# Scores in one place from slot 46, five banks for the turns and batch 0's mixing, its low-rank sum in PSUM, and the MLP from slot 56

## The chip, the cores and the metric

The kernel runs on one core of a Trainium2 chip. The metric is the device time of one execution in microseconds (us). Instructions are named by engine: TensorE (PE), VectorE (DVE), ScalarE (ACT), GpSimd (POOL) and SyncE (SP), which issues DMAs. Each engine takes its own instructions in order and waits on semaphores.

## The reference

Attention over 4 batches, 8 heads, 576 positions and head size 64, with rotary positions, is followed by a token mixing of rank 32 and an MLP over channels, everything in float32.

```
scores = (rot(q) @ rot(k).T) / sqrt(64)
attn   = exp(scores - max) / (sum + 1e-9)
x      = attn @ v                       # (4, 576, 512), heads side by side
u      = x + V.T @ (U.T @ x)            # over positions, rank 32
out    = u + relu(u @ w_ch1) @ w_ch2    # 512 -> 2048 -> 512
```

## The kernel before

**Number format.** Matmuls run in a rounded float32 format. To keep precision an operand is split into a rounded upper half and the rest (pth and ptl, xh and xl, uth and utl, hth and htl, w1h and w1l), and the products of the halves are summed. ScalarE makes the upper halves, VectorE or GpSimd the rest.

**Slots.** Work goes in slots n, one for each tile of scores (160 tiles: 32 heads of 5 tiles, the fifth with 64 rows), and 17 slots more. All engines walk through the same slots; the order in each is written out by hand. In slot n TensorE makes the scores of tile n (L881), VectorE their negated row maximum (L743), ScalarE the exponential (L606). TensorE then transposes ("turns") exponentials of earlier tiles into PSUM (L908 for the tail keys, L915 for the rest, five small ones for a head's last tile), ScalarE rounds them into pth or, for a head with its buffer there, into uth (L617), VectorE writes the rest (L752, L756). The product with v of head g-1 (L895) runs in two halves, in slots that `pv_of` gives; ScalarE copies its lower part to low (L623), VectorE adds it into xt (L766).

**Mixing.** `MIX_ALONE` says in which slot of the next batch's stretch each step of batch 0's mixing is put (s = n - 40), `MIX_MERGED` the same for the others. Steps are: natural (x turned back and scaled: L927 TensorE, L790 VectorE, then ScalarE's xh L631 and GpSimd's xl L526), low (U times x, two matmuls L937 and L938 into a bank, which VectorE copies, L803, or adds, L806, into hsum), hidden (ScalarE copies hsum to hs, L636; VectorE the rest, L810), residual (L943, VectorE L814), turned_u (L949, ScalarE L641, VectorE L818).

**MLP.** Steps of an up product (two parts of six matmuls, L967) and a down product (three parts of three matmuls, L985) are given to slots by `parts_by_slot`, from costs in the code, so that each of the `REGIONS` has a fixed number of parts. The first two steps' weights are rounded at slot `PRIME` (L648) and their rests made by GpSimd (L532); SyncE loads the first three steps' weights at slot PRIME - 3. What is left after the last slot follows in one run.

**Two orders.** Up to slot `MERGED` = 59 the mixing of slot n is done in slot n by TensorE, and in slot n + 1 by VectorE and ScalarE; scores alternate between banks 0-1 and 2-3. From slot 59 all engines do slot n's work in slot n, scores have one place (banks 0-1), so TensorE's scores wait for the exponential of the slot before, banks 2 to 4 gather the down products, bank 5 is the up product's, and turns, products with v and mixing share banks 6 and 7. Before slot 59 these share the ring of banks 4 to 7. `bank_plan` hands out banks in the order of the work; whoever takes a bank waits until the last tenant has been read (`_release`). From slot `EARLY` = 52 turns follow their scores by one slot, before by two.

## Time and profile before

| | us |
|---|---|
| median of 3 runs | 784.0 (782.77 to 784.78) |
| profiled execution | 786.62 |
| its span | 784.8 |
| TensorE busy | 716.6 |
| VectorE busy | 407.5 |
| ScalarE busy | 439.2 |
| GpSimd busy | 461.2 |

The span runs from the first to the last instruction of the profile. Busy time counts an instruction from its start to its end; matmuls overlap their predecessors' ends, so the start-to-start distance is a matmul's price in a stream. Line numbers are those of the kernel above. A slot begins on TensorE with four matmuls of L881.

### The profile page before, as it was taken

What the parts mean: (1) busy time and instruction counts of PE and PEld (TensorE: products, weight loads), DVE (VectorE), ACT (ScalarE), POOL (GpSimd) and SP (SyncE); (2) the same over time, 40 slices, a digit from 0 to 9 for tenths busy, and PEclk for the clock granted to TensorE, in tenths of its full rate; (3) what the DMA queues carried; (4) which work ended last, traced back from release to release, by engine and by line L of the source; (5) the groups of instructions that cost most, each with busy time, mean ns of one, the idle gap of its engine ahead of it and who ended that gap; (6) DMA issues with size and microseconds to landing.
All of it is one profiled execution on the core that took longest, in us unless ns stands there. A gap on an engine that the chain in (4) does not pass through costs nothing.

```text
span 784.8 us, 12208 instructions
## 1 busy us (share of the span) xinstructions
PE 716.6 (91%) x4252; PEld 643.5 (82%) x4252; DVE 407.5 (52%) x669; ACT 439.2 (56%) x944; POOL 461.2 (59%) x334
## 2 busy tenths in 40 slices
PE   0599988789999989999999999999999699999998
PEld 0588876579999777989898988889999579899896
DVE  2489997655555776444354456675555642112111
ACT  1578885557566665555465555666665333333332
POOL 2848867157767673485584866647523226556553
PEclk9989998989999999999999999999999999999999
DMA  7957761826474535728548266282623135445442
GB/s 224 224 145 191 197 181 61 237 102 154 160 182 174 147 115 169 233 75 204 174 140 232 92 176 178 89 235 74 175 69 119 41 128 164 133 160 167 129 162 80
DMA packets 74700, 119.59 MB, mean 152 GB/s; under 512 B 27152, under 2 KB 27280, under 8 KB 72848
## 3 DMA queue, kind: packets, MB, share of 16 engines
q1 hardware_dynamic: 73600, 116.98, 51.0%
q10 hardware_dynamic: 1040, 1.84, 0.8%
q8 instruction: 35, 0.57, 0.3%
q14 instruction: 25, 0.20, 0.1%
HBM read 81.04 MB, written 9.44 MB: 115 GB/s over the span
## 4 chain that ended last, share of the span: by engine, by line
PE 71%; DVE 10%; ACT 6%; issue 5%; DMA 4%; POOL 3%; SPq 1%; ACTq 0%; POOLq 0%; DVEq 0%
PE ps L967 23%; PE ps L985 22%; PE ps L895 8%; PE ps L881 8%; PE ps L915 6%; DVE negmax L743 2%; ACT prob L606 2%; DMA stack<-raw 1%; PE ps L908 1%; DVE ptl L752 1%; PE ps L949 1%; POOL raw L489 1%; DVE pth L756 1%; DMA tables<-in_sin 1%; DMA res<-in_v 1%
## 5 line engine op out<-in xcount | busy, mean ns | idle before, releaser
L532 POOL TENSOR_TENSOR w1l<-w1u,w1h 128x512 fp32r<-128x512 f32 x96 | 123.9, 1291 | 243.3 <-ACT w1h L648 243.2
L743 DVE TENSOR_REDUCE negmax<-ps 128x1 f32<-128x576 f32 (+1 forms) x160 | 120.4, 752 | 74.3 <-PE ps L881 71.4
L827 DVE SCALAR_TENSOR_TENSOR htl<-ps,hth 128x384 fp32r<-128x384 f32 x96 | 53.5, 557 | 191.3 <-ACT hth L659 191.2
L881 PE MATMUL ps<-stack 128*128 128x288 f32 (+1 forms) x640 | 120.5, 312 | 32.2 <-DMA stack<-raw 22.5
L606 ACT ACTIVATE prob<-ps,negmax 128x576 f32<-128x576 f32 (+1 forms) x160 | 117.9, 737 | 46.0 <-DVE negmax L743 43.3
L617 ACT ACTIVATE pth<-ps 128x512 fp32r<-128x512 f32 x162 | 90.9, 565 | 82.0 <-PE ps L915 80.2
L967 PE MATMUL ps<-uth,w1h 128*128 128x384 f32 x384 | 133.1, 347 | 0.5 <-DVE utl L818 0.5
L881 PEld LDWEIGHTS ps<-stack 128*128 128x128 f32 (+1 forms) x640 | 97.7, 185 | 43.6 <-issue 22.8
L659 ACT ACTIVATE hth<-ps 128x384 fp32r<-128x384 f32 x96 | 47.1, 491 | 150.5 <-PE ps L967 150.3
L967 PE MATMUL ps<-utl,w1h 128*128 128x384 f32 x384 | 129.8, 338 | 0.0
L967 PE MATMUL ps<-uth,w1l 128*128 128x384 f32 x384 | 129.8, 338 | 0.0
L538 POOL TENSOR_TENSOR w2l<-w2u,w2h 128x512 fp32r<-128x512 f32 x96 | 123.8, 1290 | 4.6 <-ACT w2h L652 4.6
L985 PE MATMUL ps<-w2h,hth 128*128 128x512 f32 x288 | 117.7, 409 | 2.1 <-DVE htl L827 1.2
L985 PE MATMUL ps<-w2l,hth 128*128 128x512 f32 x288 | 114.1, 396 | 0.0
L985 PE MATMUL ps<-w2h,htl 128*128 128x512 f32 x288 | 113.8, 395 | 0.0
L915 PE MATMUL ps<-ident,prob 128*128 128x128 f32 (+1 forms) x672 | 96.6, 269 | 10.5 <-DVE xt L766 4.0
L752 DVE TENSOR_TENSOR ptl<-ps,pth 128x512 fp32r<-128x512 f32 (+1 forms) x135 | 85.7, 636 | 32.6 <-ACT pth L617 30.9
L915 PEld LDWEIGHTS ps<-ident,prob 128*128 128x128 f32 (+1 forms) x672 | 76.7, 143 | 18.5 <-issue 18.4
L489 POOL TENSOR_TENSOR raw<-raw,tables 128x1152 f32<-128x1152 f32 x30 | 80.2, 2675 | 16.5 <-DVE raw L725 13.4
L895 PE MATMUL ps<-pth,v 128*128 128x288 f32 x270 | 78.8, 314 | 3.1 <-DVE utl L818 1.5
L967 PEld LDWEIGHTS ps<-uth,w1h 128*128 128x128 f32 x384 | 72.9, 190 | 4.2 <-issue 1.5
L967 PEld LDWEIGHTS ps<-utl,w1h 128*128 128x128 f32 x384 | 72.8, 190 | 2.8
(68 smaller groups left out, 1093.9 us busy)
## 6 DMA issues: line engine op xcount, KB each, us to landing
w1u<-in_w SPq DMA_DIRECT2D x96, 256.0 KB, 2.7
w2u<-in_w SPq DMA_DIRECT2D x96, 256.0 KB, 2.7
stack<-raw SPq DMA_DIRECT2D x64, 288.0 KB, 4.5
raw<-in_qk SPq DMA_DIRECT2D x14, 1152.0 KB, 5.5
stack<-raw SPq DMA_DIRECT2D x60, 144.0 KB, 4.2
v2u<-in_v SPq DMA_DIRECT2D x16, 320.0 KB, 3.9
res<-scratch_u SPq DMA_DIRECT2D x18, 256.0 KB, 3.8
out<-res SPq DMA_DIRECT2D x18, 256.0 KB, 2.2
```

Of the source, the lines that this page charges most:

```text
L489: link(nc.gpsimd.tensor_tensor(both, both, tables[:, :, which], ALU.mult))
L532: nc.gpsimd.tensor_tensor(w1l[:, at], w1u[:, at], w1h[:, at], ALU.subtract).then_inc(w1_lo, 1)
L538: nc.gpsimd.tensor_tensor(w2l[:, at], w2u[:, at], w2h[:, at], ALU.subtract).then_inc(w2_lo, 1)
L606: nc.scalar.activation(tile_of(n, WT[t]).rearrange("p (c n) -> p c n", c=2), scores_of(n, WT[t]), ACT.Exp, bias=negmax[0:WT[t], t:t + 1], ...
L617: nc.scalar.activation(pt_of(g)[0][rows, keys, queries], source, ACT.Copy).then_inc(pt_hi, 1)
L743: nc.vector.tensor_reduce(negmax[0:WT[t], t:t + 1], scores_of(n, WT[t]), AX.XY, ALU.max, negate=True).then_inc(maxed, 1)
L752: nc.vector.tensor_tensor(ptl[:, :, queries], source[:, full], pth[:, full, queries], ALU.subtract).then_inc(pt_lo, 1)
L881: mm = nc.tensor.matmul(ps[0:WT[t], at + c * BANK:at + c * BANK + CH], stack[:, g % HEADS_STACKED, 0, P * t:P * t + WT[t]], stack[:, g % H ...
L895: mm = nc.tensor.matmul(work(tenant, 0, P, CH), v2[:, (g // 2) % 2, kt, g % 2], part[:, kt, CH * c:CH * c + CH], start=(kt, part) == produ ...
L915: mm = nc.tensor.transpose(bank[:, c], prob[0:rows, S * first + P * c:S * first + P * c + P], ident[0:rows, 0:rows])
L967: mm = nc.tensor.matmul(up_bank(), l[:, i % WBUF, P * d:P * d + P], r, start=(d == 0 and q == 0), stop=(d == DB - 1 and q == 2))
L985: mm = nc.tensor.matmul(acc_bank(t), l[:, i % 2, P * t:P * t + P], r[:, i % WBUF], start=(f == 0 and q == 0), stop=(f == FB - 1 and q == 2))
```

## The change

`MERGED` and `EARLY` go to 46, and a new `MLP_FROM` = 56 takes over what the MLP's start needs: the first region, `PRIME` (55) and the two-bank ring. So slots 46 to 55 run in the second order (scores in one place, mixing in its own slot on all engines) without MLP parts, with a ring of five banks, `RING_MIXED` = (4, 6, 7, 2, 3), whose count starts anew at 46. Bank 5 holds batch 0's low-rank sum: the ten matmuls of its five low steps form one accumulation, VectorE's copy and four additions for batch 0 go, and hidden reads the bank instead of hsum. The first up product waits for hidden's end instead of the last tenant of bank 5. `MIX_ALONE` is put anew over slots 46 to 57, and the products with v of heads 8 to 10 move to slots 47 and 48, 50 and 52, and 55 and 57 (before: 48 and 49, 53 and 54, 56 and 58). The first region holds the same 77 MLP parts in 37 slots.

```diff
--- before.py
+++ after.py
@@ -32,25 +32,25 @@
 LOWS = UNITS + 1
 
 
-EARLY = 52
-MERGED = 59
+EARLY = 46
+MERGED, MLP_FROM = 46, 56
 PT_TWO = 9
-PV_EARLY = {3: 0, 4: 1}
-PV_ALONE = {1: 0, 3: 1}
+PV_ALONE = {3: 0, 4: 1}
+PV_SWITCH = {2: 0, 3: 1}
 PV_MERGED = {0: 0, 2: 1}
 
-MIX_ALONE = {6: [("natural", 0)],
-             7: [("natural", 1), ("natural", 2)],
-             8: [("natural", 3)],
-             9: [("natural", 4), ("low", 0)],
-             10: [("low", 1), ("low", 2)],
-             11: [("low", 3), ("low", 4)],
-             12: [("hidden", 0)],
-             14: [("residual", 0)],
-             15: [("residual", 1), ("residual", 2)],
-             16: [("residual", 3), ("turned_u", 0)],
-             17: [("residual", 4), ("turned_u", 1), ("turned_u", 2)],
-             18: [("turned_u", 3), ("turned_u", 4)]}
+MIX_ALONE = {6: [("natural", 0), ("natural", 1)],
+             7: [("natural", 2)],
+             8: [("natural", 3), ("low", 0), ("low", 1)],
+             9: [("natural", 4), ("low", 2)],
+             10: [("low", 3), ("low", 4)],
+             11: [("hidden", 0)],
+             12: [("residual", 0)],
+             13: [("residual", 1), ("turned_u", 0)],
+             14: [("residual", 2), ("turned_u", 1)],
+             15: [("residual", 3), ("turned_u", 2)],
+             16: [("residual", 4), ("turned_u", 3)],
+             17: [("turned_u", 4)]}
 MIX_MERGED = {3: [("natural", 0)], 4: [("natural", 1), ("low", 0)], 5: [("natural", 2), ("low", 1)],
               6: [("natural", 3), ("low", 2)], 7: [("natural", 4), ("low", 3)], 8: [("low", 4)], 9: [("hidden", 0)],
               10: [("residual", 0)], 11: [("residual", 1), ("turned_u", 0)], 12: [("residual", 2), ("turned_u", 1)],
@@ -83,11 +83,11 @@
         PARTS += [("up", _i + 1, 0), ("up", _i + 1, 1)]
     PARTS += [("down", _i, _t) for _t in range(TT)]
 
-REGIONS = ((59, 93, 77), (93, 134, 237), (134, NTILES, 297), (NTILES, SLOTS, 317))
-PRIME = MERGED - 1
+REGIONS = ((56, 93, 77), (93, 134, 237), (134, NTILES, 297), (NTILES, SLOTS, 317))
+PRIME = MLP_FROM - 1
 POOL_ROUNDS = range(1, 6)
 
-RING_ALONE, RING_MERGED = (4, 5, 6, 7), (6, 7)
+RING_ALONE, RING_MIXED, RING_MERGED = (4, 5, 6, 7), (4, 6, 7, 2, 3), (6, 7)
 ACC, UP = (2, 3, 4), 5
 
 
@@ -102,7 +102,8 @@
 def pv_of(n):
 
     g, t = divmod(n, NT)
-    halves = PV_EARLY if n < NT * -(-EARLY // NT) else PV_ALONE if n < MERGED else PV_MERGED
+    first = NT * (MERGED // NT)
+    halves = PV_ALONE if n < first else PV_SWITCH if n < first + NT else PV_MERGED
     return [(g - 1, halves[t])] if 1 <= g <= NHEADS and t in halves else []
 
 
@@ -157,11 +158,16 @@
         turned = [("turned", *x) for x in turned_in(n)]
         tenants = tenants + turned if n < MERGED else turned + tenants
         tenants += [("mix", *x) for x in mixes_of(n) if x[1] != "hidden"]
-        if n == MERGED:
-            left = {b: holder[b] for b in (ACC[2], UP)}
+        if n == MLP_FROM:
+            left = {b: holder[b] for b in ACC}
+        if n in (MERGED, MLP_FROM):
             count = 0
-        ring = RING_ALONE if n < MERGED else RING_MERGED
+        ring = RING_ALONE if n < MERGED else RING_MIXED if n < MLP_FROM else RING_MERGED
         for tenant in tenants:
+            if tenant[0:3] == ("mix", 0, "low"):
+                if tenant[3] == 0:
+                    bank[tenant], before[tenant] = UP, holder.get(UP)
+                continue
             b = ring[count % len(ring)]
             count += 1
             bank[tenant], before[tenant] = b, holder.get(b)
@@ -200,7 +206,7 @@
         eng.wait_ge(e["pv_out"], 2 * i + rest[0] + 1)
     else:
         read = {"natural": "x_nat", "low": "h_sum", "residual": "u_ready", "turned_u": "ut_lo"}[rest[0]]
-        eng.wait_ge(e[read], i * NT + rest[1] + 1)
+        eng.wait_ge(e[read], i * NT + rest[1] + 1 - (NT if rest[0] == "low" else 0))
 
 
 def _down_read(eng, i, e):
@@ -306,6 +312,10 @@
          "pv_low pv_out sums_eps sums_inv nat_done x_nat x_hi x_lo x_rest low_done h_sum h_hi h_ready res_done "
          "u_ready u_stored turn_done ut_hi ut_lo w1_loaded w2_loaded w1_hi w1_lo w2_hi w2_lo up_done relu_hi "
          "relu_lo down_done acc_done added res_loaded stored").split())
+
+    def hidden_of(b):
+
+        return hsum[:, :] if b else ps[:, UP * BANK:UP * BANK + DM]
 
     def scores_of(n, rows):
         at = 2 * BANK * (n % 2 if n < MERGED else 0)
@@ -630,10 +640,12 @@
                         act.wait_ge(low_done, k - XBUF + 1)
                     nc.scalar.activation(xh[0:WT[t], k % XBUF], xn[0:WT[t], t], ACT.Copy).then_inc(x_hi, 1)
                 elif what == "hidden":
-                    act.wait_ge(h_sum, NT * (b + 1))
                     if b:
+                        act.wait_ge(h_sum, NT * b)
                         act.wait_ge(res_done, NT * b)
-                    nc.scalar.activation(hs[:, :], hsum[:, :], ACT.Copy).then_inc(h_hi, 1)
+                    else:
+                        act.wait_ge(low_done, NT)
+                    nc.scalar.activation(hs[:, :], hidden_of(b), ACT.Copy).then_inc(h_hi, 1)
                 elif what == "turned_u":
                     act.wait_ge(turn_done, k + 1)
                     if b >= 2:
@@ -794,20 +806,21 @@
                                             .broadcast_to([rows, H, D]), ALU.mult).then_inc(x_nat, 1)
                     if b == B - 1:
                         split_x(b, t)
+                elif what == "low" and b == 0:
+                    pass
                 elif what == "low":
                     dve.wait_ge(low_done, k + 1)
                     part = work(("mix", b, what, t), 0, P, DM)
                     if t == 0:
-                        if b:
-                            dve.wait_ge(h_ready, b)
+                        dve.wait_ge(h_ready, b)
                         nc.vector.tensor_copy(hsum[:, :], part).then_inc(h_sum, 1)
                     else:
-                        dve.wait_ge(h_sum, k)
+                        dve.wait_ge(h_sum, k - NT)
                         nc.vector.tensor_tensor(hsum[:, :], part, hsum[:, :], ALU.add).then_inc(h_sum, 1)
                 elif what == "hidden":
                     dve.wait_ge(h_hi, b + 1)
                     third = slice(2 * R, 3 * R)
-                    nc.vector.tensor_tensor(hs[third, :], hsum[third, :], hs[third, :],
+                    nc.vector.tensor_tensor(hs[third, :], hidden_of(b)[third], hs[third, :],
                                             ALU.subtract).then_inc(h_ready, 1)
                 elif what == "residual":
                     dve.wait_ge(res_done, k + 1)
@@ -920,7 +933,9 @@
                 if what == "hidden":
                     return
                 k, rows, tenant = b * NT + t, WT[t], ("mix", b, what, t)
-                _release(pe, before[tenant], e)
+                sums_here = b == 0 and what == "low"
+                if not sums_here or t == 0:
+                    _release(pe, before[tenant], e)
                 if what == "natural":
                     pe.wait_ge(pv_out, 2 * H * (b + 1))
                     for c in range(PAIRS):
@@ -934,9 +949,11 @@
                         pe.wait_ge(x_rest, t + 1)
                     else:
                         pe.wait_ge(x_lo, k + 1)
-                    nc.tensor.matmul(work(tenant, 0, P, DM), us[0:rows, t], xh[0:rows, k % XBUF], start=True, stop=False)
-                    mm = nc.tensor.matmul(work(tenant, 0, P, DM), us[0:rows, t], xl[0:rows, k % XBUF],
-                                          start=False, stop=True)
+                    part = hidden_of(b) if sums_here else work(tenant, 0, P, DM)
+                    nc.tensor.matmul(part, us[0:rows, t], xh[0:rows, k % XBUF],
+                                     start=not sums_here or t == 0, stop=False)
+                    mm = nc.tensor.matmul(part, us[0:rows, t], xl[0:rows, k % XBUF],
+                                          start=False, stop=not sums_here or t == NT - 1)
                     mm.then_inc(low_done, 1)
                 elif what == "residual":
                     pe.wait_ge(h_ready, b + 1)
@@ -955,7 +972,7 @@
                 if part == 0:
                     pe.wait_ge(w1_lo, i + 1)
                     if i == 0:
-                        _release(pe, left[UP], e)
+                        pe.wait_ge(h_ready, 1)
                     else:
                         pe.wait_ge(relu_lo, i)
                     if f == 0:
@@ -977,8 +994,6 @@
                 if f == 0:
                     if p:
                         pe.wait_ge(added, TT * (p - 1) + t + 1)
-                    elif ACC[t] < RING_ALONE[0]:
-                        pe.wait_ge(expd, MERGED)
                     else:
                         _release(pe, left[ACC[t]], e)
                 for q, (l, r) in enumerate(((hth, w2h), (htl, w2h), (hth, w2l))):
```

## Rows read from the trace of the kernel before

**Rows 1.** The page, its first line.
```profile
span 784.8 us, 12208 instructions
```

**Rows 2.** Windows: start:end, length, then busy us (instructions) of each engine, clock, DMA.
```profile
60.00:100.00 40.00, 38.01 (x296) 35.72 (x295) 38.21 (x66) 35.75 (x84) 33.92 (x24) 1.00 0.72 191
107.91:143.86 35.95, 28.34 (x167) 22.63 (x165) 27.29 (x47) 23.26 (x50) 19.37 (x13) 0.89 0.46 119
164.04:256.17 92.13, 92.13 (x574) 85.52 (x572) 50.45 (x85) 61.69 (x137) 66.13 (x45) 0.98 0.51 149
256.17:295.76 39.59, 35.53 (x220) 30.00 (x218) 28.22 (x44) 24.29 (x52) 27.66 (x19) 1.00 0.46 130
160.00:164.00 4.00, 1.55 (x8) 1.43 (x9) 2.31 (x5) 0.43 (x1) 1.19 (x1) 0.52 0.11 42
```

**Rows 3.** TensorE's timeline in slots 70 and 71: start, length, what.
```profile
205.30 0.40 PE L895 MATMUL ps<-pth,v 128*128 128x288 f32 x1
...
206.59 0.34 PE L967 MATMUL ps<-uth,w1h 128*128 128x384 f32 x1
...
208.68 0.69 PE L881 MATMUL ps<-stack 128*128 128x288 f32 x4
209.20 0.60 PE L915 MATMUL ps<-ident,prob 128*128 128x128 f32 x4
209.56 0.48 PE L985 MATMUL ps<-w2h,hth 128*128 128x512 f32 x1
```

**Rows 4.** TensorE's timeline, slots 46 to 60; in brackets the idle time before and its releaser.
```profile
107.91 0.77 PE L881 MATMUL ps<-stack 128*128 128x288 f32 x4
108.70 0.49 PE L915 MATMUL ps<-ident,prob 64*128 64x64 f32 x5
...
110.22 0.76 PE L881 MATMUL ps<-stack 128*128 128x288 f32 x4
...
113.57 0.77 PE L881 MATMUL ps<-stack 128*128 128x288 f32 x4
...
122.53 0.63 PE L915 MATMUL ps<-ident,prob 128*128 128x128 f32 x4 [1.30 <-DVE xt L766]
...
143.86 1.17 PE L881 MATMUL ps<-stack 128*128 128x288 f32 x4
...
162.45 1.08 PE L915 MATMUL ps<-ident,prob 128*128 128x128 f32 x4 [2.83 <-DVE utl L818]
...
164.04 0.67 PE L967 MATMUL ps<-uth,w1h 128*128 128x384 f32 x1
...
167.58 0.69 PE L881 MATMUL ps<-stack 128*128 128x288 f32 x4
```

**Rows 5.** VectorE's timeline, slots 46 to 52.
```profile
111.05 0.68 DVE L756 TENSOR_TENSOR pth<-ps,pth 64x512 fp32r<-64x512 f32 x1
...
114.38 0.76 DVE L743 TENSOR_REDUCE negmax<-ps 128x1 f32<-128x576 f32 x1 [0.56 <-PE ps L881]
...
118.29 0.44 DVE L766 TENSOR_TENSOR xt<-ps,low 64x288 f32<-64x288 f32 x1
...
127.64 1.49 DVE L806 TENSOR_TENSOR hsum<-ps,hsum 128x512 f32<-128x512 f32 x2
```

**Rows 6.** ScalarE's timeline, slot 48.
```profile
115.17 0.74 ACT L606 ACTIVATE prob<-ps,negmax 128x576 f32<-128x576 f32 x1 [0.20 <-DVE negmax L743]
...
116.03 0.41 ACT L623 ACTIVATE low<-ps 64x288 f32<-64x288 f32 x1
...
117.62 0.60 ACT L617 ACTIVATE uth<-ps 128x512 fp32r<-128x512 f32 x1
```

**Rows 7.** GpSimd's timeline, slots 47 to 51.
```profile
114.56 1.29 POOL L526 TENSOR_TENSOR xl<-xn,xh 128x512 fp32r<-128x512 f32 x1 [2.00 <-ACT xh L631]
...
122.73 2.66 POOL L489 TENSOR_TENSOR raw<-raw,tables 128x1152 f32<-128x1152 f32 x1
125.47 1.40 POOL L490 TENSOR_TENSOR raw<-raw 128x576 f32<-128x576 f32 x1
```

## The prediction

> **What bounds the kernel now.** I read the page first, then the windows by stretch, then TensorE's timeline slot by slot (each slot begins with its four score matmuls), and then the timelines of VectorE, ScalarE and GpSimd from slot 46 to 59. The span is 784.8 us [rows 1]; the execution took 786.62, and the three timed runs have a median of 784.0. So I make the sum as a difference and take it from 784.0. Three regimes show in [rows 2]. Attention alone (60 to 100 us) is bound by VectorE, busy 38.2 of 40 us; its 296 matmuls, at 63 for a head of five slots, are 23.5 slots, 1.7 us each. Once the MLP's parts are spread between the scores, TensorE has no gap: 92.13 busy of 92.13 us, and its order of instructions is the bound. Between them lie slots 46 to 58, batch 0's mixing, where nothing is full: 28.3 of 35.95 us busy on TensorE and 27.3 on VectorE in slots 46 to 55 (and the busy TensorE includes stretches at half clock, 0.89 granted on average). That is 3.6 us a slot, over twice the 1.7; 20.2 us more pass from there to the first MLP matmul at 164.04 [rows 4]. Since TensorE is the bound afterwards, the end comes when the MLP begins plus TensorE work left over; time saved or lost up to there goes nearly one for one to the end.
>
> Why the middle is slow is seen in TensorE's waits [rows 4]. At 122.53 it has idled 1.30 us for VectorE's addition into xt, at 162.45 2.83 us for VectorE's utl. These are bank releases. With a ring of four banks, the bank that the turns of slot 50 need was last held by an attention product; VectorE adds that only after the row maximum of slot 50, and this needs the scores that TensorE has just made. So each slot runs TensorE, VectorE, TensorE in series. At 162.45 it is the step to the two-bank ring at slot 59, which must wait for batch 0's last turned tile.
>
> **Prices, from the rows.** TensorE's stream is read from start to start [rows 3]: scores 0.52 (208.68 to 209.20), turns 0.36 (to 209.56), attention product 1.29 (205.30 to 206.59), an up pair 2.09 (206.59 to 208.68). From the scores' start to the maximum's it is 0.81 (113.57 [rows 4], 114.38 [rows 5]). VectorE [rows 5]: row maximum 0.76, a split, natural, residual or turned-u step 0.68 (0.60 back to back), xt addition 0.44. ScalarE [rows 6]: exponential 0.74, with its accumulator read 0.86 (115.17 to 116.03), rounding 0.60, low 0.41. GpSimd [rows 7]: xl 1.29, a rope 2.66 + 1.40.
>
> **The change, part by part.** *Low-rank sum in PSUM.* It removes one copy and four additions of 128x512, by [rows 5] 0.75 each (1.49 for two), about 3.7 us of VectorE. This engine is on the chain, but the last two already lay in the wait for hidden, so I count it only through the schedule below. ScalarE's and VectorE's reads of hidden change from SBUF to PSUM; the same shapes from PSUM take 0.60 and 0.68, so nothing changes there. TensorE's ten matmuls are the same. In front of the residual the up bank is free anyhow.
>
> *Scores in one place, from slot 46.* A slot's scores now wait for the exponential of the slot before. The bare loop is scores 0.81 until the maximum begins, 0.76, exponential 0.86 and handing on: 2.5 us, and 2.7 with the rounding that now stands ahead of the exponential. That is more than 1.7 and less than 3.6, so it is hidden unless mixing is already quick. The Trainium skill (Perfetto Trace Analysis, Optimizing Tensor Performance, Matmuls) has independent groups rotate through banks so that one's evacuation lies beside the next one's matmuls. By that rule scores in one place cost, and a fifth bank for the turns gains; the trace agrees on the second (the 1.30 us wait at 122.53), and on scores no row here shows the one place without MLP parts between. That is the rival with the long loop, below.
>
> *Order.* From slot 46 VectorE and ScalarE do the mixing of slot n in slot n, no longer a slot later. So behind a natural step of slot n queue the row maximum of n+1, and behind ScalarE's xh the next rounding and exponential. This is the real price.
>
> I laid the slots out from 107.91, scores of 46 [rows 4], with these prices, 0.03 to 0.05 a handing on, at full clock. Slot 46: the new ring gives the five small turns of head 8 bank 4 (it was bank 5), whose holder, the tail turn, is split by VectorE at 111.05 for 0.68 [rows 5]. TensorE, which went on at 108.70, now waits until 111.8. Rounding ends 112.76, the exponential 113.6, so slot 47's scores start 113.65, where they started 110.22: 3.4 us lost at once. 47: first the xh of naturals 0 and 1, then rounding, exponential (118.1). 48: natural 2's xh holds ScalarE to 120.2, exponential to 121.6, TensorE's two lows to 121.95. 49: scores 121.95, exponential to 125.2. 50: the tail's split ends 126.4, the product follows; natural 4 at 127.0, xh 127.6, xl (1.29) 128.9, the last low 129.5. 51: scores 129.5, exponential to 132.2. Then ScalarE wants head 12's rope, whose 4.1 us on GpSimd [rows 7] follow that last xl: 133.0; its copy, hidden's copy and split end at 135.0. 52: maximum only then, exponential to 136.65. 53: to 139.8. 54: to 143.3. 55: to 147.3, with residuals and turned tiles in them. Slot 56 begins at 147.35 against 143.86: **3.5 us later**.
>
> *MLP from slot 56.* The two first weight splits now stand at slot 55: w1h 148.3, w1l 149.6; the third turned tile is split at 150.2. The six loads go out ahead of head 12's value load and stacks on SyncE and wait for nothing, so they hold nothing up and are long in. So the first up part runs at 150.25, 13.8 us ahead of 164.04 [rows 4]. Behind it one wait comes back: in slot 57 the product of head 10 needs bank 6, held by turned tile 3, to 155.85, and the turn of 58 waits until 158.35. After that TensorE has work always. By then it has done 2.1 us of MLP and owes 1.8 us of slots 58 and 59, so it stands where before stood at 164.04 if it were 158.05: **6.0 us gained** (9.5 of it here, less the 3.5).
>
> *Clock.* Before 164.04 the granted clock was 0.52 (nearly all of it the lower level, 1.2 GHz) after 1.55 busy of 4 us [rows 2], and the twelve up matmuls from 164.04 to 167.58 [rows 4] took 3.5 us where 2.09 is their price. I expect the same at 150.3, after two thin slots: it shifts the wait of slot 57 by about 1.7, against the 1.45 paid before: 0.3 lost, and 0.3 more after the 3.4 us pause in slot 46. Half-clock stretches inside 46 to 55, which the 35.95 us hold and my layout doesn't, and slips in handing on: between 0 and 4; I take **1.0**, since the chain there runs mostly through VectorE and ScalarE, whose durations don't follow this clock.
>
> *The MLP's spread.* The same 77 parts now lie in 37 slots instead of 34; from slot 93 on the plan is the same. Slots 84 to 92 get some 1.4 us less to do between batch 1's mixing, where TensorE is idle for 4.1 of 39.6 us already [rows 2]. If those slots are held by their chains, up to 1.4 us are lost; if not, none: 0.7.
>
> Sum: 6.0 - 0.3 - 0.3 - 1.0 - 0.7 = **3.7 us**, 784.0 - 3.7 = **780.3 us**.
>
> **Rivals.** *The long loop (slower).* If mixing in the same slot costs more than I laid out, slots 46 to 55 eat the gain. Those ten cost 3.94 us each in my layout and 0.1 in reserve; at 4.4 nothing is left, and at 4.7, as when one more step of VectorE's 0.68 lies in the chain of each, the end is 3 us later: 787. For it speaks that 3.4 us go in slot 46 alone; against it that five banks take the waits of 1.3 us away. It decides if slot 56's scores start after 152 (147.35, the 3.7 and the 1.0 in reserve). 0.15.
>
> *Washed out (no change).* The gain is made, but stalls in slots 57 to 60 or in batch 1's mixing take it: slot 57's bank wait of 1.7 once more in slots 58 and 59, or all 1.4 us there. Time 782.5 to 784.5. 0.20.
>
> *More gained.* The clock stays up, mixing 46 to 55 is as quick as before (35.95 us): 3.5 + 1.0 + 0.6 more, at most 8.8 gained, 775.2. 0.13. The forecast itself, a gain of 2.4 to 6 us: 0.52.
>
> **Numbers.** Less than 0.3% (2.4 us) can't be told from no change by a measurement of this kernel. Faster 0.65, within 0.20, slower 0.15. The range takes 775.5 to 785.8: the low end is the great gain, the high end the washed-out case and the first part of the long loop.
>
> **What would show it.** After: TensorE idles some 3 us in slot 46 for VectorE's split of the tail; slots 47 to 55 have no wait for xt, but VectorE's maximum begins late, behind natural, residual and turned steps; hsum has no row for batch 0; slot 56's scores start near 147 to 149, the first up matmul near 150 to 152, and one wait for utl stands in slot 57. From slot 58 TensorE has no gap until batch 1's mixing, and slot 93 begins some 4 us earlier than at 295.76. I'd be wrong if the first up matmul stood later than 155, if slots 57 to 60 idled over 4 us, or if batch 1's stretch grew by more than 1.5 us over 39.59.

## The result and the profile after

The changed kernel took 773.25 us (771.76 to 774.56, 4 runs) against 783.56: a ratio of 0.987 (95% interval 0.9839 to 0.9901), 10.3 us less. It was run again in two later blocks (a block is a series of runs made together, with the kernel before in it): 775.21 us against 783.69, ratio 0.9891 (0.9867 to 0.9916), and 775.67 against 783.53, ratio 0.9905 (0.9875 to 0.9935). So the medians put the gain at 7.9 to 10.3 us, and the first block is the largest. The execution profiled there, 771.76 us, is the fastest of its four, with a mean granted clock of 0.996 where the other three had 0.987 to 0.989. The forecast was 3.7 us less, 780.3, with a range down to 775.5. The direction was right and the size was not; the two later medians lie near the range's low end.

The page's first line, of after:

```profile
span 770.0 us, 12193 instructions
```

The spans differ by 14.8 us [rows 1], but 4.74 of these are no work of the change: slot 46's scores start at 103.17 instead of 107.91 [rows 4]. Up to there both kernels do the same; the first scores came 1.66 us sooner, and TensorE ran at half clock from 37.4 to 44.0 us in the profile of before, not in that of after. So I count from slot 46's scores. From there to the end of the span it is 676.9 us before and 666.8 after.

TensorE's timeline of after in slots 46 to 58; in brackets the idle time before, and its releaser (L894 scores, L928 turns, L908 product with v, L984 up, L960 residual, L953 low):

```profile
103.17 0.77 PE L894 MATMUL ps<-stack 128*128 128x288 f32 x4
107.13 1.08 PE L928 MATMUL ps<-ident,prob 64*128 64x64 f32 x9 [3.19 <-DVE pth L768]
108.05 1.04 PE L942 MATMUL ps<-ident,xt 128*128 128x128 f32 x8
108.87 0.80 PE L894 MATMUL ps<-stack 128*128 128x288 f32 x4
...
113.15 0.80 PE L894 MATMUL ps<-stack 128*128 128x288 f32 x4 [1.42 <-ACT prob L616]
...
120.27 0.76 PE L894 MATMUL ps<-stack 128*128 128x288 f32 x4 [1.00 <-ACT prob L616]
...
124.10 0.49 PE L953 MATMUL ps<-xh,us 64*128 64x512 f32 x1 [0.74 <-POOL xl L536]
...
127.40 0.80 PE L894 MATMUL ps<-stack 128*128 128x288 f32 x4 [1.41 <-ACT prob L616]
...
130.22 0.46 PE L960 MATMUL ps<-hs,vs 128*128 128x512 f32 x1 [0.37 <-DVE hs L823]
131.78 0.80 PE L894 MATMUL ps<-stack 128*128 128x288 f32 x4 [1.10 <-ACT prob L616]
...
134.94 0.75 PE L894 MATMUL ps<-stack 128*64 128x288 f32 x4 [0.81 <-ACT prob L616]
...
138.34 0.77 PE L894 MATMUL ps<-stack 128*128 128x288 f32 x4 [1.10 <-ACT prob L616]
...
142.29 0.79 PE L894 MATMUL ps<-stack 128*128 128x288 f32 x4 [0.67 <-ACT prob L616]
...
145.20 0.41 PE L984 MATMUL ps<-uth,w1h 128*128 128x384 f32 x1 [1.68 <-DVE utl L831]
...
150.59 0.40 PE L908 MATMUL ps<-pth,v 128*128 128x288 f32 x1 [1.41 <-DVE utl L831]
...
152.36 0.82 PE L894 MATMUL ps<-stack 128*128 128x288 f32 x4
```

These answer to [rows 4]. Slot 47 begins 5.70 us after slot 46 (before 2.31), behind a wait of 3.19 us for VectorE's split of the tail turn. From slot 48 to 56 seven of nine slots begin with a wait for ScalarE's exponential, 0.67 to 1.42 us. The waits for xt of [rows 4] are gone from slots 47 to 55; in slots 56 and 57 there are waits for utl, 1.68 us ahead of the first up matmul and 1.41 in slot 57, where before waited 2.83 in slot 59. Slot 56 begins 39.12 us after slot 46, the first up matmul 42.03.

Windows of after: slots 46 to 55, then from slot 59 to the end of slot 83 nearly (158.5 to 246), then slots 84 to 92; start:end, length, busy us of each engine, granted clock:

```profile
103.17:142.29 39.12, 27.06 (x189) 22.70 (x186) 27.21 (x48) 23.86 (x53) 19.49 (x14) 1.00 0.61 171
158.50:246.00 87.50, 86.73 (x548) 79.76 (x546) 49.54 (x83) 57.78 (x130) 62.44 (x42) 1.00 0.51 154
246.05:281.48 35.43, 33.96 (x212) 28.98 (x213) 26.67 (x44) 24.61 (x52) 26.06 (x19) 1.00 0.48 138
```

Against [rows 2], the mixing's window is 3.2 us longer, at a granted clock of 1.00 instead of 0.89. Batch 1's mixing, slots 84 to 92, is 35.43 us long instead of 39.59.

To compare slots with different MLP parts in them I take, for each slot's start, the time from slot 46's scores and subtract the MLP parts done since, at 1.045 us an up part (half of the 2.09 of [rows 3]) and 0.70 a down part. What then differs is idle time or matmuls at half clock:

```
                        slot 56   slot 60   slot 93
before                    35.95     57.58    122.91
before, second profile    36.27     58.90    124.39
after                     39.12     49.73    113.37
after, second             40.24     50.85    114.53
after, third              39.14     51.32    115.00
```

The gain by slot 60 is 7.85 us in the first pair, by slot 93 9.54. Over all pairs of a profile of before and one of after it is 6.3 to 9.2 us by slot 60 and 7.9 to 11.0 by slot 93. In the first pair TensorE, from slot 46 to 60, is busy for 44.82 us and idle for 14.85 before, and busy for 41.89 and idle for 15.16 after. Less the MLP parts (2.09 and 7.32 us) its busy time fell by 8.2 us and its idle time rose by 0.3: the gain shows as matmuls that did not run at half clock, not as fewer gaps. After slot 93 both run the same plan; what differs there between profiles of one kernel (486.7 and 489.1 us from slot 93 to the end for before) is as large as what differs between the kernels.

### The profile page after: what moved, and what is told of

Its sections match the earlier page's. It is cut to its first block, busy times and chain, and to the rows that moved or that the text cites. A ratio compares the mean times of both kernels' runs of the same rounds, so it can differ in the third digit from the quotient of the medians.

```text
span 770.0 us, 12193 instructions
## 1 busy us (share of the span) xinstructions
PE 707.1 (92%) x4252; PEld 636.0 (83%) x4252; DVE 404.4 (53%) x664; ACT 438.8 (57%) x944; POOL 461.2 (60%) x334
## 4 chain that ended last, share of the span: by engine, by line
PE 68%; DVE 9%; ACT 8%; issue 5%; POOL 4%; DMA 4%; SPq 1%; ACTq 0%; POOLq 0%; DVEq 0%
PE ps L984 23%; PE ps L1000 22%; PE ps L894 7%; PE ps L908 7%; PE ps L928 5%; DVE negmax L755 3%; ACT prob L616 2%; POOL raw L499 1%; PE ps L921 1%; DMA stack<-raw 1%; DMA tables<-in_sin 1%; DVE pth L768 1%; DMA res<-in_v 1%; DVE utl L831 1%; PE ps L966 1%
## 5 line engine op out<-in xcount | busy, mean ns | idle before, releaser
L894 PE MATMUL ps<-stack 128*128 128x288 f32 (+1 forms) x640 | 118.2, 307 | 37.8 <-DMA stack<-raw 20.8
L894 PEld LDWEIGHTS ps<-stack 128*128 128x128 f32 (+1 forms) x640 | 95.0, 181 | 51.7 <-issue 24.9
L984 PE MATMUL ps<-uth,w1h 128*128 128x384 f32 x384 | 132.6, 345 | 2.2 <-DVE utl L831 2.2
L984 PE MATMUL ps<-uth,w1l 128*128 128x384 f32 x384 | 129.8, 338 | 0.0
L984 PE MATMUL ps<-utl,w1h 128*128 128x384 f32 x384 | 129.5, 337 | 0.0
L928 PE MATMUL ps<-ident,prob 128*128 128x128 f32 (+1 forms) x672 | 93.7, 264 | 3.3 <-DVE pth L768 3.2
L928 PEld LDWEIGHTS ps<-ident,prob 128*128 128x128 f32 (+1 forms) x672 | 75.2, 140 | 9.2 <-issue 8.9
L908 PE MATMUL ps<-pth,v 128*128 128x288 f32 x270 | 77.4, 310 | 3.2 <-DVE utl L831 3.0
L984 PEld LDWEIGHTS ps<-uth,w1h 128*128 128x128 f32 x384 | 72.6, 189 | 6.1 <-POOL w1l L542 1.9
L984 PEld LDWEIGHTS ps<-utl,w1h 128*128 128x128 f32 x384 | 72.6, 189 | 3.3
```

The costliest lines, as they stand in the source:

```text
L894: mm = nc.tensor.matmul(ps[0:WT[t], at + c * BANK:at + c * BANK + CH], stack[:, g % HEADS_STACKED, 0, P * t:P * t + WT[t]], stack[:, g % H ...
L908: mm = nc.tensor.matmul(work(tenant, 0, P, CH), v2[:, (g // 2) % 2, kt, g % 2], part[:, kt, CH * c:CH * c + CH], start=(kt, part) == produ ...
L928: mm = nc.tensor.transpose(bank[:, c], prob[0:rows, S * first + P * c:S * first + P * c + P], ident[0:rows, 0:rows])
L984: mm = nc.tensor.matmul(up_bank(), l[:, i % WBUF, P * d:P * d + P], r, start=(d == 0 and q == 0), stop=(d == DB - 1 and q == 2))
```

## The experiments

Half-clock stretches come and go between profiles of one kernel, so a run's main reading is its distance between slots, with the stretches in it; it comes from one profile. The time is named beside it. Edits are against the changed kernel where nothing else is said.

**Both kernels again.** No edit.

> The kernel before, unchanged, for a second profile. What it decides is how much of the 14.9 us between the two spans belongs to the change. 4.7 us of it are there already at slot 46, ahead of anything that the change touches: the first scores 1.66 us earlier, and a half-clock stretch from 37 to 44 us that the changed kernel's profile lacks. Theory A (chance): this profile may lack the early stretch too, and the distance from slot 46 to slot 93 is again 187.9 us, half-clock stretches in slots 52 to 59 included, because these follow from the long idle stretches on TensorE there. Rival B: the half-clock stretches between slots 46 and 59 are chance as well; then a profile without them shows 183 to 185 us from slot 46 to 93 and part of the gain was luck of one profile.

> The changed kernel, unchanged, for a second profile and a closer ratio. Theory A: from slot 46 to slot 93 178.3 us again, within 0.5, with no half-clock stretch there, since its waits are spread thin. Rival B: a half-clock stretch falls in slots 46 to 60 in this execution and the distance is 180 to 182 us. Ratio near 0.987 (0.985 to 0.989).

> The changed kernel once more, beside the same blocks as the three others of this call. From slot 46 to 93 178.3 us plus 1.1 for a half-clock stretch at slot 46's pause and 1.6 for one where the MLP begins, if they fall in this execution: so 178.3, 179.4, 180.0 or 181. Time 773 to 775.5.

Before, second profile: 782.2 us, an early half-clock stretch again (36.1 to 39.6), 189.3 us from slot 46 to 93 where theory A had 187.9 again, with half-clock stretches at 124.9 to 131.7, 138.5 to 145.4 and 159.0 to 165.8. Rival B (183 to 185 us without them) did not come: both profiles of before have three such stretches in slots 50 to 60. The changed kernel gave 775.21 and 775.67 us and 179.5 and 179.9 us to slot 93: one stretch right behind the pause of slot 46 in both, costing 1.12 us at slot 56 in the second and nothing in the third, and one at the MLP's beginning in the third alone. So theory A of the second profile (178.3 us and no stretch) was wrong, and the third's 179.95 is one of the sums expected of it. The third profile in windows: slots 46 to 55, the stretch at the MLP's beginning, and the one behind the pause:

```profile
107.21:146.35 39.14, 28.47 (x189) 24.23 (x186) 27.34 (x48) 23.88 (x53) 19.41 (x13) 0.96 0.62 171
149.30:152.70 3.40, 3.40 (x11) 3.21 (x12) 1.77 (x3) 1.46 (x3) 0.53 (x1) 0.50 0.41 149
111.80:115.20 3.40, 3.40 (x17) 3.38 (x16) 2.46 (x5) 2.05 (x5) 0.00 (x0) 0.50 1.00 229
```

The granted 0.50 is the lower level, 1.2 GHz. Slot 57 then begins 7.23 us after slot 56, without it (in the first profile) 5.66: 1.57 us.

**The MLP at slot 59 again.**

```diff
-MERGED, MLP_FROM = 46, 56
+MERGED, MLP_FROM = 46, 59
-REGIONS = ((56, 93, 77), (93, 134, 237), (134, NTILES, 297), (NTILES, SLOTS, 317))
+REGIONS = ((59, 93, 77), (93, 134, 237), (134, NTILES, 297), (NTILES, SLOTS, 317))
```

> The changed kernel, with the MLP entering at slot 59 again (first region, weights and two-bank ring at 59, five banks up to 58). Theory A, the schedule by hand: slots 56 to 58 then pass in 3.0 to 3.5 us each with TensorE mostly idle, the first up matmul stands at 48 to 51 us after slot 46's scores (before: 56.1, changed: 42.0), and the kernel is 3 to 5 us slower than the changed one: 776.5 to 778.5. Rival B, the mixing itself holds the path and MLP parts in 56 to 58 only lengthen it: within 1 us of the changed kernel.

777.59 us, ratio 0.9931 (0.9907 to 0.9956). Slots 56 to 58 took 3.64, 3.37 and 2.83 us, the first up matmul stood at 50.8 and slot 60 at 53.03 us after slot 46. On the scale above it is at 50.94 at slot 60 (changed 49.73, before 57.58). Neither this profile nor the first of after has a half-clock stretch from slot 46 to 60, so of the 7.85 us only 1.2 need the MLP from 56. Theory A's places were about right, its 3 to 5 us were not: the kernel is 2.4 us slower than the changed one of its block, and it also has the old parts in slots 84 to 92 (40.3 us, with a half-clock stretch in them).

**The mixing late, too.** `MLP_FROM` = 59 with its first region, as in the run before, and the residual and turned steps of `MIX_ALONE` in their old slots:

```diff
...
-             12: [("residual", 0)],
-             13: [("residual", 1), ("turned_u", 0)],
-             14: [("residual", 2), ("turned_u", 1)],
-             15: [("residual", 3), ("turned_u", 2)],
-             16: [("residual", 4), ("turned_u", 3)],
-             17: [("turned_u", 4)]}
+             14: [("residual", 0)],
+             15: [("residual", 1), ("residual", 2)],
+             16: [("residual", 3), ("turned_u", 0)],
+             17: [("residual", 4), ("turned_u", 1), ("turned_u", 2)],
+             18: [("turned_u", 3), ("turned_u", 4)]}
```

> The changed kernel with the MLP at slot 59 and residual and turned steps in their old slots 54 to 58 (1, 2, 2, 3, 2 steps instead of 2 a slot from 52 on); order, five banks, PSUM sum stay. It tells what made slots 56 to 59 take 23.7 us before and 13.9 in the run with the MLP at 59. Theory A (the order and the rings: VectorE a slot late, and the step to two banks in slot 59): slot 60 begins at 53 to 56 us after slot 46 here too (before: 59.7). Rival B (the bunching of turned steps in slots 57 and 58): 58 us or more.

779.27 us (0.9956, 0.9934 to 0.9978); slot 60 begins at 58.13. Rival B. TensorE's timeline in slot 59 (L893 scores, L927 turns, L983 up):

```profile
158.25 1.22 PE L893 MATMUL ps<-stack 128*64 128x288 f32 x4 [2.17 <-ACT prob L615]
160.93 1.09 PE L927 MATMUL ps<-ident,prob 128*128 128x128 f32 x4 [1.45 <-DVE utl L830]
...
162.52 0.67 PE L983 MATMUL ps<-uth,w1h 128*128 128x384 f32 x1
162.99 0.52 PE L983 MATMUL ps<-utl,w1h 128*128 128x384 f32 x1
```

Here TensorE waits 2.17 us for the exponential and 1.45 for utl, where [rows 4] have one wait of 2.83 us for utl. On the common scale slot 60 stands at 56.04, 1.5 us ahead of before. Against the run with the MLP at 59 it is 5.1 us later, and this difference isn't the schedule's alone. Two half-clock stretches lie in this run, in windows of its profile; the third row and the one below it are slots 46 to 59, here and in the run with the MLP at 59:

```profile
137.70:147.90 10.20, 8.78 (x35) 7.49 (x36) 5.51 (x11) 5.17 (x12) 1.79 (x2) 0.50 0.67 153
158.10:164.90 6.80, 5.19 (x19) 4.59 (x20) 3.05 (x5) 3.69 (x10) 2.50 (x2) 0.50 0.32 127
107.65:165.78 58.13, 42.01 (x256) 36.43 (x254) 37.13 (x64) 33.39 (x73) 23.39 (x16) 0.85 0.57 161
```
```profile
108.02:161.05 53.03, 37.01 (x256) 31.27 (x253) 36.98 (x64) 33.86 (x73) 23.44 (x16) 1.00 0.62 175
```

The same 256 matmuls take 5.0 us more of TensorE's time, and it is idle for as long (16.12 and 16.02 us). Such time is lost in part only: in the second and third profiles of after the half-clock stretches lengthen TensorE's busy time to slot 60 by 2.6 and 3.0 us and bring slot 60 1.1 and 1.6 us later. By that share, an estimate, the clock made 2.1 to 2.7 of the 5.1 us and the late steps the other 2.4 to 3.0. Each side is one profile, and the medians of the two runs, in different blocks, are 1.7 us apart. All four profiles with the late steps (before twice, before with new MLP parts, and this one) have about 17 us or more at half clock from slot 46 to 60, the twelve with the early steps 0 to 14 us. So the two go together; that the late steps bring the half clock is not shown.

**Five banks, one place.** The ring (4, 6, 7, 2); and scores in two places until slot 56 with the ring (4, 6, 7):

```diff
-RING_ALONE, RING_MIXED, RING_MERGED = (4, 5, 6, 7), (4, 6, 7, 2, 3), (6, 7)
+RING_ALONE, RING_MIXED, RING_MERGED = (4, 5, 6, 7), (4, 6, 7, 2), (6, 7)
```

```diff
-RING_ALONE, RING_MIXED, RING_MERGED = (4, 5, 6, 7), (4, 6, 7, 2, 3), (6, 7)
+RING_ALONE, RING_MIXED, RING_MERGED = (4, 5, 6, 7), (4, 6, 7), (6, 7)
...
-        at = 2 * BANK * (n % 2 if n < MERGED else 0)
+        at = 2 * BANK * (n % 2 if n < MLP_FROM else 0)
-                if n > MERGED:
+                if n > MLP_FROM:
```

> The changed kernel, with a ring of four banks (4, 6, 7, 2) in slots 46 to 55 instead of five. Theory A (what removed the 1.3 us waits is that VectorE reads a slot's banks in that slot, not the fifth bank): slot 56 begins within 1 us of 39.1 us after slot 46, time within 1 us. Rival B, my prediction's reading (the fifth bank takes the waits away): TensorE waits for releases again in slots 47 to 54, slot 56 begins 2 us or more later.

> The changed kernel, with scores alternating between two places in slots 46 to 55, and so only three banks (4, 6, 7) in the ring. Theory A (VectorE and ScalarE, each doing the slot's mixing in order, set the pace, and scores wait only because ScalarE's exponential is late): the earlier scores are read no sooner, slot 56 begins between 1 us earlier and 2 us later than 39.1. Rival B, the long loop (the one place costs): 2 us or more are gained, TensorE's 1.0 to 1.4 us waits for the exponential go, VectorE's maximum follows them earlier. Rival C: three banks bring waits of 1 us for releases in most slots, and it is 3 us or more slower.

Four banks: slot 56 at 39.14 us, ratio 0.9904 (0.9868 to 0.9941). Two places and three banks: 39.28, ratio 0.9879 (0.9831 to 0.9927). Theory A in both. With two places slot 52 begins 1.6 us sooner (22.59), and by slot 56 waits of 0.3 to 0.8 us for VectorE's steps have eaten it. Neither the fifth bank nor the one place moves the mixing's end by more than 0.2 us. No run has the old order of work alone from slot 46 on, so what the order gives by itself is not measured.

**The low-rank sum by VectorE again.**

```diff
-                if tenant[3] == 0:
-                    bank[tenant], before[tenant] = UP, holder.get(UP)
-                continue
...
-        return hsum[:, :] if b else ps[:, UP * BANK:UP * BANK + DM]
+        return hsum[:, :]
...
-                elif what == "low" and b == 0:
-                    pass
```

> The changed kernel, with batch 0's low-rank sum undone alone: five low steps take banks of the ring again, VectorE copies the first and adds the other four into hsum, hidden reads hsum. Theory A (the engines' order in a slot is what counts): 5 steps of 0.6 to 0.75 us of VectorE come back in slots 48 to 50, ahead of the row maxima, and nearly all is on the path: slot 56 begins 42 to 43 us after slot 46 instead of 39.1 and the kernel takes 2.5 to 3.7 us more. Rival B (in slots 48 and 50 ScalarE and GpSimd hold the path, VectorE has room): under 1.5 us more.

776.38 us (0.9905, 0.9875 to 0.9935), slot 56 at 41.47: 2.35 us later, between rival B's 1.5 and the 2.9 to 3.9 of theory A's 42 to 43, with three half-clock stretches in it, so that the schedule's own share is not known closely. One part of it I had not counted. VectorE's timeline: hidden's split with hsum as operand in this run, with the bank in the changed kernel, and GpSimd's rope product beside each:

```profile
133.05 1.89 DVE L816 TENSOR_TENSOR hs<-hsum,hs 32x512 fp32r<-32x512 f32 x1 [1.39 <-ACT hs L642]
```
```profile
131.73 2.66 POOL L495 TENSOR_TENSOR raw<-raw,tables 128x1152 f32<-128x1152 f32 x1
```
```profile
129.38 0.69 DVE L823 TENSOR_TENSOR hs<-ps,hs 32x512 fp32r<-32x512 f32 x1 [2.03 <-ACT hs L648]
```
```profile
128.10 2.65 POOL L499 TENSOR_TENSOR raw<-raw,tables 128x1152 f32<-128x1152 f32 x1
```

Both splits were reached while GpSimd was in its product. That with two operands in SBUF took 1.89 us and ended at 134.94, 0.55 after the product's end at 134.39; that with its operand in PSUM took 0.69 and ended in the middle of the product.

**The MLP parts beside batch 1's mixing.** The changed kernel with the old parts in slots 84 to 92, and the kernel before with the new ones:

```diff
-REGIONS = ((56, 93, 77), (93, 134, 237), (134, NTILES, 297), (NTILES, SLOTS, 317))
+REGIONS = ((56, 84, 62), (84, 93, 77), (93, 134, 237), (134, NTILES, 297), (NTILES, SLOTS, 317))
...
+FIXED = {84: 1, 85: 1, 86: 2, 87: 1, 88: 2, 89: 3, 90: 1, 91: 3, 92: 1}
...
-            while done < end and (n == last - 1 or spent + part_ns(PARTS[done]) / 2 < goal * (n - first + 1)):
+            while done < end and (done - start < FIXED[n] if n in FIXED else
+                                  n == last - 1 or spent + part_ns(PARTS[done]) / 2 < goal * (n - first + 1)):
```

In the kernel before the first region is cut at 84 with 63 parts, and `FIXED` holds 2, 0, 2, 1, 2, 3, 1, 2, 1.

> The changed kernel, with the MLP parts of slots 84 to 92 as before the change (1, 1, 2, 1, 2, 3, 1, 3, 1 instead of 2, 0, 2, 1, 2, 3, 1, 2, 1). Between slots 84 and 93 the changed kernel gained about 3.1 us on its parts, where I had put a loss of 0.7. Theory A: the gain comes from which parts stand there (none in slot 85, one less in 91), so it is given back here: the stretch from 84 to 93 becomes 39 to 39.6 us, TensorE again waits 1.4 us for the second split of turns in slot 90, and the kernel takes 1.5 to 2.5 us more than the changed one. Rival B: it comes from the earlier arrival (other DMA phase, weights further ahead); then the stretch stays 1.5 us or more under 39 and the time is that of the changed kernel within 0.6.

> The kernel before, with nothing changed but the MLP's parts in slots 84 to 92 (2, 0, 2, 1, 2, 3, 1, 2, 1 as in the changed kernel, 63 instead of 62 ahead of 84). Theory A (which parts stand beside batch 1's mixing is what gained 2 us there): 84 to 93 falls from 39.6 to 35.4 us, 1.5 us of parts done less, 0.7 of it before 84, and the whole is 1.9 us faster than before: 780.5 to 782.5. Rival B (the state in which slot 84 is reached matters too): the stretch stays above 37 us.

With the old parts: 39.60 us from slot 84 to 93, and slot 93 1.9 us later than in the third profile of after, which has the same two half-clock stretches. But the time, 775.03 us (0.9889, 0.9865 to 0.9914), is that of the changed kernel of the same block (775.21): theory A's 1.5 to 2.5 us more are seen in the slots and not in the medians. With the new parts in the kernel before: 35.36 us, slot 93 2.8 us sooner, 780.6 us, ratio 0.9968 (0.9946 to 0.999). The stretch follows the parts, whatever came before it: theory A on this point. VectorE's hidden step in the kernel before (L810), with its GpSimd neighbour, and in after (L823) with its own:

```profile
281.97 2.85 DVE L810 TENSOR_TENSOR hs<-hsum,hs 32x512 fp32r<-32x512 f32 x1
```
```profile
281.62 2.65 POOL L489 TENSOR_TENSOR raw<-raw,tables 128x1152 f32<-128x1152 f32 x1
```
```profile
269.79 1.50 DVE L823 TENSOR_TENSOR hs<-hsum,hs 32x512 fp32r<-32x512 f32 x1
```
```profile
268.07 2.67 POOL L499 TENSOR_TENSOR raw<-raw,tables 128x1152 f32<-128x1152 f32 x1
```

2.85 us and 1.50, both ending 0.55 us after the rope product's end. With the new parts VectorE comes to the step 1.7 us after the product has begun instead of 0.35. To see whether the product holds it:

```diff
-                link(nc.gpsimd.tensor_tensor(both, both, tables[:, :, which], ALU.mult))
+                    for part in range(2):
+                        link(nc.gpsimd.tensor_tensor(both[:, part], both[:, part], tables[:, part, which], ALU.mult))
```

(for slot 90's rope alone, with the old parts; then for slots 90 and 130, in the kernel with bank 5 below.)

> The changed kernel with the old MLP parts in slots 84 to 92, and GpSimd's rope product of slot 90 (128x1152, 2.65 us) cut into two of 128x576. Theory A (VectorE's hidden step, both operands in SBUF, can't start while a GpSimd instruction runs, and starts when that one ends): it starts at the end of the first half and lasts 1.5 to 1.8 us from its entry instead of 2.85; slots 84 to 93 take 38.2 to 38.8 us instead of 39.6. Rival B (it is slow for another reason, such as the traffic to the same tiles): 2.8 us again and 39.6.

> The kernel with slot 46's small turn in bank 5, and the rope products of slots 90 and 130 cut in two likewise. Theory A: batch 1's hidden step loses little (it had 1.5 us; the second half ends where the whole did, so 1.5 or less), batch 2's falls from 2.84 to 1.6 us, and from slot 93 to 134 up to 1 us is gained, if TensorE waited for it there. Time 0 to 1.5 us under the run with bank 5 alone (771 to 772.6). Rival B: nothing moves.

```profile
274.82 1.60 DVE L832 TENSOR_TENSOR hs<-hsum,hs 32x512 fp32r<-32x512 f32 x1
```

GpSimd's first half in that run:

```profile
274.44 1.42 POOL L506 TENSOR_TENSOR raw<-raw,tables 128x576 f32<-128x576 f32 x1
```

1.60 us instead of 2.85, ending 0.56 us after the first half's end, and slots 84 to 93 38.35 instead of 39.60: the instruction of GpSimd holds it, and the hold costs 1.25 us there. (One run, 777.24 us.) The new parts make the stretch 35.43, with one up part (1.05 us) fewer in it, so the hold is 1.25 of 3.1 us. The rest also follows the parts, for the waits listed on TensorE in slots 84 to 92 sum to 3.8 us with the old ones and to 1.3 with the new, but no run takes them apart.

With halves in slots 90 and 130 batch 2's step fell from 2.84 to 1.60 us, as theory A had it, and slot 130 took 5.71 us instead of the 6.39 of the kernel with bank 5 alone, whose TensorE waited 0.42 there for VectorE's pth. Batch 1's step came in the second half and took 1.78 us, not the 1.5 or less expected. The kernel took 772.29 us (0.9864, 0.9839 to 0.9889), no less than without: 0.7 us are seen in slot 130 and not in the median.

**Slot 46's small turn in bank 5.**

```diff
-            b = ring[count % len(ring)]
-            count += 1
+            if tenant == ("turned", MERGED // NT - 1, LAST):
+                b = UP
+            else:
+                b = ring[count % len(ring)]
+                count += 1
```

and the ring in the order (6, 7, 2, 3, 4).

> The changed kernel, with one thing in the bank plan altered: the small turn of head 8 in slot 46 goes to bank 5 (free at that time), and the ring begins (6, 7, 2, 3, 4), so that it no longer waits for the split of the tail turn. Theory A (slot 46's 3.2 us wait is on the path): slot 47 begins 3.3 to 4.0 us after slot 46 instead of 5.7, and 1.5 us or more of it last to slot 56 (37.6 or less instead of 39.1); the kernel is 1.5 to 2.2 us faster than the changed one, near 772. Rival B: VectorE, with two splits and two naturals in slot 46, sets slot 47's maximum anyway; slot 48 begins within 0.5 us of 10.0 us, and nothing is gained.

> The kernel with slot 46's small turn in bank 5, once more. In its first profile slot 56 began at 37.53 us (changed: 39.12), and a half-clock stretch at the MLP's first parts took 1.6 us again. Theory A: that stretch is chance (it was there in 3 of 6 profiles of this schedule), so here slot 93 begins 176.7 us after slot 46 without it and 178.3 with it, and the median lies 1 to 2 us under the changed kernel's of this call. Rival B: an earlier start calls the stretch out each time, and the gain is paid back: 178.3 again, medians equal within 0.7 us.

772.63 us (0.9867, 0.9837 to 0.9898) and, beside the changed kernel's 775.67 in the same block, 771.33 (0.9841, 0.9816 to 0.9866). Slot 47 begins 4.01 us after slot 46, slot 56 37.53. In the first run a half-clock stretch at the MLP's beginning took the 1.6 us back (slot 93 at 178.33), in the second there was none (176.77): theory A. Of the 4.3 us between the medians of that block the slots explain 1.6; that the rest is the clock and scatter is argued. It has the lowest median here.

## Why the prediction was wrong in size

*What bounds it, and where gains go*: right. From slot 60 to 83 TensorE works almost without gaps in both kernels (after: 86.7 of 87.5 us), and what was gained ahead stays there, but for 0.55 us (7.30 left at slot 83). Slot 83 takes another 0.9, 0.56 of it in a wait for the exponential: 6.43 at slot 84.

*The slots by hand*: right, nearly to the slot. Slot 47 at 5.70 after slot 46 (I had 5.74), slot 56 at 39.12 (39.44), the first up matmul at 42.03 (42.34), slot 58 at 49.19. No slot start up to 56 is off by over 0.45 us in this profile; in the second slot 56 stands at 40.24, behind a half-clock stretch. By the same working the measured slots would have given 6.5 us instead of 6.0. The wait for the tail's split, for head 12's rope ahead of hidden, and slot 57's wait for turned tile 3 (1.41) all stand where I put them.

*Clock*: the term of the sum that was mis-sized first. By the prediction's terms slot 60 stood at 6.0 - 0.3 - 0.3 - 1.0 = 4.4 us gained; the first pair of profiles shows 7.85. The first profile of after has no half-clock stretch between slots 46 and 93. So the 1.45 us that before pays in slot 59 were gained, where I had a net loss of 0.3 (1.75), slot 46's pause took no 0.3, and the reserve of 1.0 wasn't used: 3.05 us, and 0.5 from the layout, against 3.45 missing. It isn't a certain gain: the second and third profiles of after have a stretch at slot 46's pause, and of all eleven profiles with the MLP from slot 56 five have one at its first parts, at 1.5 to 2.0 us, near the 1.7 that I had priced, and a sixth one in slot 58. What is steady is that the three stretches in each profile of before became none to two in those of after. That the first one of after had none was luck; but even the least favourable pair of profiles gives 6.3 us by slot 60, over my 4.4. By the share reckoned for the late mixing, an estimate, the 8.2 us of busy time that went are worth 3.5 to 4.4 of the 7.85. Why the stretches left is open: TensorE's idle time did not shrink (14.85 and 15.16 us).

*The MLP's spread*: the step that failed, with the wrong sign. I had up to 1.4 us lost "if those slots are held by their chains" and put 0.7. Measured from slot 60 to 93 were 1.7 us gained in the first pair: 1.4 lost ahead of slot 84 and 3.1 gained in slots 84 to 92, which have one up part (1.05 us) less to do, not 1.4. In the kernel before the new parts alone gave 2.8. With the 3.45 above this makes the 5.8 us between my 3.7 and the 9.54. Those slots are held by a chain, but its length isn't fixed. It depends in part (1.25 us) on when VectorE arrives at hidden, because a GpSimd instruction that runs at that time holds it. I took durations as fixed; this one is 0.68, 1.50 or 2.85 us by its neighbour.

*Low-rank sum in PSUM*: "nothing changes there" was wrong for hidden's split, 0.69 instead of 1.89 us. That the copy and additions lay on the path was right: 2.35 us by slot 56, the hold of 1.2 us and three half-clock stretches among it.

*MLP from slot 56*: the 9.5 us were found, the reason was not. Only 1.2 us need the MLP's entry, for slots 56 to 58 also pass quickly without it (3.64, 3.37 and 2.83 us). 5.1 came with the residual and turned steps being over two slots sooner and two a slot, so that they don't pile up in slots 57 to 59; by the estimate above 2.4 to 3.0 of them are these steps' and the others the clock's. The last 1.5 came with the order, the banks and the low-rank sum.

*Scores in one place, five banks*: the fifth bank, which I held against the long loop, does nothing for slot 56 (39.14 against 39.12). The waits of 1.3 us stayed away with four banks and with three, so it is not their number; that they went because VectorE reads a slot's banks in the slot is the reading left, and no run tests it alone. The Trainium skill (Perfetto Trace Analysis, Optimizing Tensor Performance, Matmuls) would have independent groups rotate through different banks; here neither more banks for the turns nor a second place for scores moved slot 56 by over 0.2 us. *The long loop* didn't happen, nor was the gain washed out. *More gained* came nearest, with 775.2 us, which my range from 775.5 left out; but it came near by luck, for its condition, slots 46 to 55 as quick as before (35.95 us), failed: they took 39.12.

## What to carry to other kernels

Lay a latency-bound stage out by hand from the rows, slot by slot: 39.44 us stood against 39.12. Keep apart what the schedule gives and what the clock gives or takes, and don't charge a clock loss to the new kernel alone when both kernels are exposed to it. When the fill of slots is moved, look which instruction with two SBUF operands on VectorE will now meet a long GpSimd instruction, and give the last tenant of a bank at a switch of rings as much thought as the first wait of the steady state.

## What the runs showed of the hardware

VectorE's subtraction of 32x512 took 0.68 or 0.69 us with GpSimd idle or with one operand in PSUM, and ended about 0.55 us after the end of GpSimd's product when both operands lay in SBUF and that product was running: 1.50, 1.89 and 2.85 us, depending on the arrival alone. The Trainium skill (SBUF — State Buffer, SBUF: two separate sides) has a VectorE operation with two SBUF inputs and a GpSimd operation that reads SBUF take turns at a shared pair of ports, each for a whole instruction; the runs agree, down to the 1.60 us when the product was cut in two. It is listed as busy time of VectorE, not as a wait.

TensorE's clock at half (1.2 GHz) came in other places in profiles of one kernel: in slots 46 to 60, three stretches in each of two profiles of before; none, one and two in the three of after. Its cost differs with the place: one at slot 46's pause moved slot 56 by 1.12 us in one profile and by nothing in another.
